# One step later for the weight work, earlier halves at a block's start, and a reordered attention end

## The reference

```python
q_p, k_p = phi(q), phi(k)                 # exp(+-(proj - max|proj|)), 256 features
kv = einsum('bhsf,bhsd->bhfd', k_p, v);  z = k_p.sum(axis=2)
attn = (q_p @ kv) / (q_p @ z + 1e-6)      # x: 2304 x 512
h = x @ w_in                              # 512 -> 2048
y = (h * clip(h + 3, 0, 6) / 6) @ w_out   # 2048 -> 512
e = argmax(y @ w_gate)                    # one of 8 experts per row
out = p[e] * sigmoid(y @ w_output_gate)[e] * (relu(y @ w1[e]) @ w2[e])
```

## Time and profile before

| what | us |
|---|---|
| median of 3 runs | 891.78 (891.55 to 892.68) |
| profiled execution, whole | 891.2 |
| its span | 889.4 |
| PE busy | 842.6 (95%) |
| DVE busy | 573.2 (64%) |
| ACT busy | 411.7 (46%) |

### The profile page before, as it was taken

The page is one execution under the profiler, slowest core; times in us unless marked ns, Lnnn a source line. Parts: engine busy times, 40 slices in busy tenths (PEclk is TensorE's granted clock), DMA queues, the critical chain, the costliest instruction groups (busy, mean ns, idle before and its releaser), DMA issues.

```text
span 889.4 us, 19938 instructions
## 1 busy us (share of the span) xinstructions
PE 842.6 (95%) x7258; PEld 563.1 (63%) x7259; DVE 573.2 (64%) x1200; ACT 411.7 (46%) x838; POOL 181.8 (20%) x207
## 2 busy tenths in 40 slices
PE   7999999997699999999999999999999999999994
PEld 5888777875355455455455455455766777777773
DVE  4777888885596987888788788864652345222221
ACT  5676577774356566565575575553301112111110
POOL 4444367751000002001001001001021222111100
PEclk9999999999999999999999999999999999999998
DMA  7345664442356365456555556256336572646610
GB/s 219 107 160 171 216 185 150 157 136 84 123 213 213 143 213 226 166 197 220 190 190 225 189 190 225 95 207 231 108 113 233 222 284 64 234 184 221 239 62 13
DMA packets 44884, 156.13 MB, mean 176 GB/s; under 512 B 7894, under 2 KB 12246, under 8 KB 38160
## 3 DMA queue, kind: packets, MB, share of 16 engines
q1 hardware_dynamic: 38896, 138.33, 43.5%
q0 software_dynamic: 5760, 16.80, 5.4%
q10 hardware_dynamic: 160, 0.07, 0.0%
HBM read 109.44 MB, written 47.47 MB: 176 GB/s over the span
## 4 chain that ended last, share of the span: by engine, by line
PE 77%; DVE 10%; issue 5%; ACT 3%; POOL 2%; DMA 1%; another core or an unknown queue 1%; DVEq 0%; POOLq 0%; ACTq 0%
PE ps L854 19%; PE ps L843 16%; PE ps L950 13%; PE ps L938 12%; PE ps L757 4%; PE ps L702 3%; PE ps L729 2%; DVE arena L1228 2%; DVE u_mx L1439 2%; ACT arena L1052 1%; POOL arena L527 1%; PE ps L928 1%; DVE y_mx L1417 1%; PE ps L716 1%; DMA arena<-in_moe_w 1%
## 5 line engine op out<-in xcount | busy, mean ns | idle before, releaser
L843 PE MATMUL ps<-arena,w_in_sb 128*128 128x384 f16 x1152 | 201.0, 326 | 1.5 <-issue 1.5
L854 PE MATMUL ps<-w_out_sb,arena 128*128 128x512 f16 x576 | 172.3, 381 | 13.5 <-DVE stage L1527 12.7
L843 PEld LDWEIGHTS ps<-arena,w_in_sb 128*128 128x128 f16 x1152 | 110.7, 98 | 75.5 <-issue 2.0
L1205 ACT ACTIVATE x_sb<-ps 128x512 f16<-128x512 f32 x54 | 31.6, 596 | 204.3 <-PE ps L938 173.8
L938 PE MATMUL ps<-x_sb,arena 128*128 128x128 f16 x2112 | 122.0, 219 | 3.2 <-issue 3.2
L938 PEld LDWEIGHTS ps<-x_sb,arena 128*128 128x128 f16 x2112 | 119.4, 98 | 7.4 <-issue 3.8
L950 PE MATMUL ps<-arena,x_sb 128*128 128x512 f16 x528 | 118.0, 379 | 2.1 <-DVE x_sb L1618 2.1
L854 PE MATMUL ps<-w_out_sb,stage 128*128 128x512 f16 x288 | 109.7, 381 | 0.0
L1174 ACT ACTIVATE arena<-relu 128x384 f16<-128x384 f32 x96 | 50.2, 523 | 118.6 <-DVE relu L1522 117.3
L1052 ACT ACTIVATE arena<-ps,arena 128x128 f32<-128x128 f32 x288 | 79.4, 382 | 54.9 <-DVE arena L1230 51.9
L854 PEld LDWEIGHTS ps<-w_out_sb,arena 128*128 128x128 f16 x576 | 55.6, 98 | 74.0 <-issue 17.5
(11 more groups left out here) (210 smaller groups left out, 1003.0 us busy)
## 6 DMA issues: line engine op xcount, KB each, us to landing
arena<-split SPq DMA_DIRECT2D x36, 1024.0 KB
arena<-in_moe_w SPq DMA_DIRECT2D x16, 2048.0 KB, 13.1
split<-arena SPq DMA_DIRECT2D x16, 2048.0 KB, 7.4
arena<-in_qkt SPq DMA_DIRECT2D x15, 576.0 KB, 6.2
stage<-in_moe_w_in SPq DMA_DIRECT2D x16, 512.0 KB, 4.3
stage<-in_moe_w_out SPq DMA_DIRECT2D x16, 512.0 KB, 5.4
x_sb<-rows POOLq DMA_DIRECT2D x27, 257.0 KB, 3.0
arena<-in_v SPq DMA_DIRECT2D x32, 128.0 KB, 4.6
```

The source lines that it names most:

```text
L843: last = nc.tensor.matmul(ps[:, HB[f % GB], 0:BN], w_in_sb[:, lw, c, f * P:(f + 1) * P], xt[:, a, c, lx, :], start=c == 0 and lw + lx == 0 ...
L854: last = nc.tensor.matmul(ps[:, YB + r, :], g_sb[lg_][:, f % GB, r * P:(r + 1) * P], w_out_sb[:, lw, f, :], start=f == 0 and lg_ + lw == 0 ...
```

## The change

It has four parts.

1. **Units one step later** (`UNIT_AT = 1`): every piece of a unit moves from step f to f + 1 on DVE and ACT. The second `unit_lo` of a block's third unit, which was in step 15, falls into step 0 of the next block.
2. **Block start.** DVE takes `row_scales` ahead of `gate_chunk(0)`, not behind `gate_lo(0)`; `gate_lo(1)` comes straight behind `gate_chunk(1)`; `rows_hi` moves from step 1 to 0 and `rows_lo` from step 3 to step 1. `Y_AT` goes from 4 to 3, and the transposes, copies, logits, ranks and routing go one step earlier with it.
3. **Attention end.** PE takes numerators 0 and 1 and the tails ahead of all four row transposes. `x_hi(0)` waits only for the scale it uses, `x_lo(0)` stands ahead of the two `piece_lo_of`, and the pieces of the last pair (with `wg_lo` and `base`) move behind the first gate of block 0. PE's wait for `x_ready` moves from ahead of `hidden(1)` to ahead of `output(0)`.
4. **POOL** does one `partition_all_reduce` into an unused tile `warm` at the end of attention.

```diff
-Y_AT, X_AT = 4, 10
+Y_AT, X_AT = 3, 10
+UNIT_AT = 1
+X_UP = 11
@@ POOL, last_pair
                 piece_hi_of(PAIRS - 1, 1)
+                nc.gpsimd.partition_all_reduce(warm[:], ones[:, 0:1], P, RMAX)
@@ PE, both
                     pe.wait_ge(pk_ready, u * 3 + 3)
-                    for c in range(2):
-                        x_transpose(0, c, X0[c])
...
                 else:
-                    for c in range(2, DC):
+                    for c in range(DC):
                         x_transpose(0, c, X0[c])
@@ PE, mlp_block
                 hidden(n, a, 0)
-                if first:
-                    pe.wait_ge(x_ready, PAIRS)
                 hidden(n, a, 1)
...
+                    if first and f == 0:
+                        pe.wait_ge(x_ready, PAIRS)
...
-                    if post and f == 9 - ahead:
+                    if post and f == Y_AT + 5 - ahead:
                         y_logits(n - 1)
@@ ACT, x_hi
-                    act.wait_ge(x_scale, 1)
+                    act.wait_ge(scale_step, X_UP)
@@ ACT, mlp_block
-                    k, j = divmod(f, 5)
-                    if k < units and j == 3:
+                    if post and f == 0:
+                        rows_hi(n - 1)
+                    k, j = divmod(f - UNIT_AT, 5)
+                    if 0 <= k < units and j == 3:
                         unit_hi(n * 3 + k, (odd + k) % 2, 0)
-                    if k < units and j == 4:
+                    if 0 <= k < units and j == 4:
                         unit_hi(n * 3 + k, (odd + k) % 2, 2)
-                    if post and f == 1:
-                        rows_hi(n - 1)
                     if post and Y_AT + 2 <= f + ahead // 2 < Y_AT + 2 + DC:
                         copy_yt(n - 1, f + ahead // 2 - Y_AT - 2, XB)
@@ DVE, values_pair and last_pair
                 x_scales()
+                x_lo(0)
                 for w in range(2):
                     piece_lo_of(u, a, w)
...
             def last_pair():
-                x_lo(0)
                 pair_out(PAIRS - 1, 1)
+
+            def last_pieces():
                 for w in range(2):
                     piece_lo_of(PAIRS - 1, 1, w)
@@ DVE, mlp_block
                 for f in range(FC):
-                    gate_chunk(n, f)
-                    if f in (0, FC - 1):
-                        gate_lo(n, f)
                     if post and f == 0:
                         row_scales(n - 1)
-                    k, j = divmod(f, 5)
+                    gate_chunk(n, f)
+                    if f in (0, 1, FC - 1):
+                        gate_lo(n, f)
+                    if f == 0 and not post:
+                        last_pieces()
+                    if f == 0 and post:
+                        unit_lo(n * 3 - 1, 1 - a, 2)
+                    if post and f == 1:
+                        rows_lo(n - 1)
+                    k, j = divmod(f - UNIT_AT, 5)
...
-                    if post and f == 3:
-                        rows_lo(n - 1)
-                    if f == 8 and units == 3:
+                    if f == 9 and units == 3:
                         x_lo(n + 1)
```

More of the change, by code:

```diff
@@ L174, in moe_program @@
         u_all = sb("u_all", [P, 2])
+        warm = sb("warm", [P, 1])
         u_pow = sb("u_pow", [P, UNITS])
@@ L914, in mlp_block @@
                         y_transpose(n - 1, f + ahead // 2 - Y_AT, XB)
-                    if post and f == 9 - ahead:
+                    if post and f == Y_AT + 5 - ahead:
                         y_logits(n - 1)
-                    if post and f == 11 - ahead:
+                    if post and f == Y_AT + 7 - ahead:
                         ranks(n - 1)
@@ L1166, in mlp_block @@
                     if isinstance(n, int) and n == 0 and f == 0:
+                        act.wait_ge(x_scale, 1)
                         act.wait_ge(pads_stored, 16 * E)
@@ L1174, in mlp_block @@
                     nc.scalar.mul(g_sb[0][:, f % GB, :], relu3[:, f % GB, :], CG / 6.0).then_inc(g_hi, 1)
-                    k, j = divmod(f, 5)
-                    if k < units and j == 3:
+                    if post and f == 0:
+                        rows_hi(n - 1)
+                    k, j = divmod(f - UNIT_AT, 5)
+                    if 0 <= k < units and j == 3:
                         unit_hi(n * 3 + k, (odd + k) % 2, 0)
-                    if k < units and j == 4:
+                    if 0 <= k < units and j == 4:
                         unit_hi(n * 3 + k, (odd + k) % 2, 2)
-                    if post and f == 1:
-                        rows_hi(n - 1)
                     if post and Y_AT + 2 <= f + ahead // 2 < Y_AT + 2 + DC:
                         copy_yt(n - 1, f + ahead // 2 - Y_AT - 2, XB)
-                    if post and f == 12 - ahead:
+                    if post and f == Y_AT + 8 - ahead:
                         gate_exp(n - 1)
@@ L1370, in last_pair @@
                                                op0=ALU.mult, op1=ALU.subtract).then_inc(wg_lo, 1)
+                dve.wait_ge(consts_made, 2)
+                nc.vector.tensor_copy(base[:, 0, :], start8[:]).then_inc(route, 1)
             def x_max():
@@ L1377, in x_scales @@
                 scales(slice(3, 4))
+                assert scale_steps[0] == X_UP + 1
                 scaled(nc.vector.tensor_tensor(s_h[:], s_inv[:, 3:4], s_inv[:, 0:1], ALU.mult))
@@ L1400, in _ @@
             last_pair()
-            dve.wait_ge(consts_made, 2)
-            nc.vector.tensor_copy(base[:, 0, :], start8[:]).then_inc(route, 1)
             def row_scales(n):
@@ L1566, in mlp_block @@
                 for f in range(FC):
-                    gate_chunk(n, f)
-                    if f in (0, FC - 1):
-                        gate_lo(n, f)
                     if post and f == 0:
                         row_scales(n - 1)
-                    k, j = divmod(f, 5)
+                    gate_chunk(n, f)
[8 more added lines that the diff above has]
+                    k, j = divmod(f - UNIT_AT, 5)
                     if j == 0 and 0 < k <= units:
                         unit_lo(n * 3 + (k - 1), (a + k - 1) % 2, 2)
-                    if j == 1 and k < units:
+                    if j == 1 and 0 <= k < units:
                         unit_search(n * 3 + k, (a + k) % 2, 0)
-                    if j == 2 and k < units:
+                    if j == 2 and 0 <= k < units:
                         unit_search(n * 3 + k, (a + k) % 2, 2)
-                    if j == 3 and k < units:
+                    if j == 3 and 0 <= k < units:
                         unit_scale(n * 3 + k, (a + k) % 2)
-                    if j == 4 and k < units:
+                    if j == 4 and 0 <= k < units:
                         unit_lo(n * 3 + k, (a + k) % 2, 0)
-                    if post and f == 3:
-                        rows_lo(n - 1)
-                    if f == 8 and units == 3:
+                    if f == 9 and units == 3:
                         x_lo(n + 1)
@@ L1588, in mlp_block @@
                         star_pick()
-                    if post and f == 11 - ahead:
+                    if post and f == Y_AT + 7 - ahead:
                         route_first(n - 1)
-                    if post and f == 13 - ahead:
+                    if post and f == Y_AT + 9 - ahead:
                         route_second(n - 1)
-                    if ahead and f == 13 - ahead:
+                    if ahead and f == Y_AT + 9 - ahead:
                         early_rows()
-                    if f not in (0, FC - 1):
+                    if f not in (0, 1, FC - 1):
                         gate_lo(n, f)
```

## The result

The changed kernel takes 881.72 us (median of 4 runs, 880.84 to 882.41) against 892.23 us for the kernel before in the same comparison (4 runs, 891.55 to 893.27): the ratio is 0.9881 with a 95% interval of 0.9864 to 0.9898, 1.2% faster. The forecast was 884.2, the range 878.0 to 889.0.

What follows compares the result with a forecast made beforehand. PE, busy 95% of the span, was taken to bound the kernel. Terms -4.4 - 8.8 + 3 x 1.2 + 0.5 + 1.7 = -7.4 from 891.2 gave 883.8, with 0.6 for the median 884.3, rounded to 884.2; range 878.0 to 889.0.

Steps and rivals of the forecast that it cites:

- Attention's end, -4.4: Attention's end: PE idles some 0.8 us instead of 4.39, hidden(0) begins at 209.1 instead of 213.53; -4.4 us.
- The bound that the clock might fall behind the short idle stretch: Attention's end: clock 0.59 behind the 0.8 us idle would add 1.1 to the first numerators and 0.6 to the transposes.
- Block 0, -8.8: Block 0: of 9.0 us of waits and low clock, all but 0.26 goes; -8.8 us.
- Blocks 1, 2 and 4, +1.2 each: DVE wait moves from step 1 to 2, gain nil; PE stands 1.2 us for ACT's copy at the transposes.
- The two waits named as signs, 1.3 and about 1.2: Blocks 1, 2 and 4: 1.3 us at output(2) for the gate, about 1.2 at the transposes for ACT's copy.
- The rival that the waits vanish: Blocks 1 to 5: DVE's queue keeps up, 5.7 us of waits go, no copy is late; 872.9 us, chance 0.12.
- Its halfway case, 878.6: Blocks 1 to 5: copy in time but T(2), output of step 2, still late; 878.6 us, counted within the 0.12 chance.
- Block 3, +0.5: Block 3, behind the loop's back branch: its wait of 0.4 goes, the copy is 0.9 late; +0.5 us.
- block 5, +1.7: Block 5, transposes one step earlier: copy of group 0 late 1.25, the next 0.2, the start 0.2; +1.7 us.
- Experts, 0: Behind block 5: last unit stored and first expert's loads some 5 us later, costed at nothing.
- The sum: All terms together: -7.4 us against the profiled execution's 891.2, giving 883.8, before 0.6 for the median.
- 2.5 us in each of four blocks: Slower-than-before rival: copy_xt of group 3 late behind unit_hi in step 15, delaying the next block's hidden(0); 893.8 us, chance 0.05.

Runs made afterwards that it cites:

- experiment 1: The kernel before plus only the unused partition reduction on POOL at attention's end: 888.90 us, ratio 0.9958.
- experiment 3: The changed kernel without the unused partition reduction on POOL: 887.44 us, ratio 0.9945 to the kernel before.
- experiment 5: The kernel before with only the MLP blocks' new order (units one step later, early block start), no attention-end change, no unused reduction: 893.40 us, ratio 1.0019.
- Experiment 4: The changed kernel with the copy of the transposed rows placed ahead of the unit's high half on ACT: 878.26 us, ratio 0.9839.
- experiment 2: The kernel before with only the attention-end part of the change: 887.11 us, ratio 0.9947.
- experiment 6: The changed kernel with rows_lo back in step 3 and the transposes one step later (Y_AT = 4): 880.38 us, ratio 0.9874.
- experiment 7: The changed kernel with rows_hi in step 1, rows_lo in step 4, transposes two steps later (one step earlier each in block 5): 879.05 us, ratio 0.9860.
- experiment 8: The changed kernel run once more, unmodified, for the spread: 881.58 us, ratio 0.9889.
- Experiment 9: The copy-first version (experiment 4) with gate_lo ahead of the search in step 2 too: 880.14 us, ratio 0.9867.
- experiment 10: The copy-first version (experiment 4) with gate_lo ahead of the search in steps 2 and 3: 883.08 us, ratio 0.9903.
- experiment 11: The copy-first version (experiment 4) with gate_lo directly behind its chunk in all sixteen steps: 925.31 us, ratio 1.0357.

## Why the prediction was right

**Attention's end, -4.4.** Between the two traces it is -4.27, and by the same steps: `x_hi` 200.96 to 202.55, numerators from 203.13, transposes from 205.68, 0.22 for bank 3, hidden(0) at 209.26 (forecast 209.1). But the near match is in part luck. Measured from the z sums the term is -4.87, so the forecast was 0.47 short, and a start 0.60 later, which the change did not make, covers that up. The bound that the clock might fall behind the short idle stretch did not come in: it was granted in full.

**Block 0, -8.8.** Measured -8.61. The load is issued at 211.24 and used at 220.40 (211.0 and 220.0 in the forecast), output(2) waits 0.29 (0.26), and POOL's gap moved in front of the unused reduction. That is 6.8 us of waits and 1.8 of lower clock. Experiments 1, 3 and 5 split this term: the reordering removes the wait for the load, the unused reduction the gap, and each leaves the other's wait standing.

**Blocks 1, 2 and 4, +1.2 each.** Measured +1.19, +0.96 (with a back branch that was 0.21 shorter) and +1.17. The layout of the queue held: output(0), (1) and (2) begin 6.14, 10.04 and 15.21 us behind hidden(0), against 5.99, 9.98 and 15.17. The copy of the transposes runs from 25.54 to 26.32 against 25.5 to 26.3. The two waits named as signs, 1.3 and about 1.2, stand in the rows as 1.12 and 0.93; the forecast counted from an undisturbed start, and the rows count PE's idle time alone. Experiment 4 removes the stall at the copy and nothing else, and the five blocks become 4.4 us shorter in spite of a back branch that was 0.9 longer; experiment 5 shows the reordering as a loss. The rival that the waits vanish (872.9) is refuted by both. Its halfway case, 878.6, is what the kernel gives once the copy is put first: 878.26.

**Block 3, +0.5, and block 5, +1.7.** Measured -0.15 and +1.43. The copy is 0.93 late in block 3, as laid out, but a 0.74 us issue wait of PE ahead of output(0), which the trace of before has in this block, is absent after. The three traces with the old order of the steps have such a wait there (0.74, and 1.02 and 1.28 in experiments 1 and 2), and none of those with the new order has. I had not read that row: this term was 0.65 too high.

**Experts, 0.** Measured -1.02. The code there is the same. Before has one wait of 2.1 us for `x_sb` (L1618) there, after has one of 1.2 for an expert's load. In the traces of experiments 1 to 10 the phase took 261.3 to 263.9 us, so a microsecond either way is scatter of this stretch and need not be the change's doing; which transfer decides it in a given execution I did not settle.

**The sum.** -7.4 was forecast and -9.3 measured between the two traces: 1.0 is the expert phase, 0.65 block 3, 0.5 attention's end, 0.3 block 5, 0.2 the back branch, against 0.6 for the later start of the z sums and 0.2 for block 0. The median lies another 0.7 below the forecast, since 0.6 was added for a median above the profiled execution, and after the change the two agree (881.72 and 881.79). No step of the forecast failed; mostly the terms put at nothing or by analogy were off. One rival has a slip: 2.5 us in each of four blocks, added to the forecast of 884.3, is 894.3 and not 893.8, which starts from the profiled execution.

The expectations of experiments 6, 7, 10 and 11 fared worse than the forecast, and mostly for one reason. The forecast time of each followed the queue of DVE with care and took ACT's to be free, though the rivals of 10 and 11 named ACT or a lack of slack. In block 1 of the changed kernel DVE's low halves of gates 1 to 3 end 0.1 to 0.7 us ahead of the outputs that need them, and ACT's copy is 0.93 late, so what is taken out of one queue appears in the other. Experiment 9 had the wait right (1.1 expected, 1.26 measured) and the time 1.8 us too low.

## What to carry to other kernels

Price a moved step on both engines that feed the critical one, from the start of the block, instruction by instruction: if the reordered queue holds as much work ahead of the same deadline, the wait only changes its place. Here the wait for DVE moved by one step at no gain, and a second one, for ACT, cost about 1.2 us in each of blocks 1, 2 and 4. Of two instructions in one step, the one that another engine waits for goes first; that change of order was worth 3.5 us, where the reordering of the steps in blocks 1 to 5 had cost 4.6. And where an engine's first instruction of a kind is preceded by a long idle gap that no semaphore explains, an unused one placed in an idle stretch takes the gap off the path: 3.4 us alone, 5.7 once it was the last long wait of its block and took the low clock with it.

## What the runs showed of the hardware

In all thirteen traces POOL's first partition reduction began 5.5 to 6.3 us behind the two instructions that set POOL up for it, in its old place (5.8 in the kernel before, 6.3 in experiment 3) and in its new one (5.8 in the changed kernel, 5.7 in experiment 1), and every later one within half a microsecond of its maxima. The Trainium skill, GPSIMD Engine Reference, section 2.1, says that the first call of a freshly loaded kernel pays a load of about 6 us. These rows agree. They also show that an unused call on a one-column tile is enough to pay it.

The back branch of the loop over blocks held PE between 1.2 and 2.3 us in all profiled executions but that of the slowest version (0.16), with the same loop in each. In four of them it was 2.11, 2.12, 2.15 and 2.26 us. Behind 2.12 (experiment 6) and 2.26 (experiment 9) the granted clock fell to its lower level of 1.2 GHz; the windows of experiment 9:

```profile
412.20:416.20 4.00, 4.00 (x15) 2.02 (x16) 1.49 (x7) 0.23 (x1) 0.00 (x0) 0.58 0.01 4
416.20:419.80 3.60, 3.60 (x24) 2.15 (x22) 2.54 (x4) 2.98 (x6) 0.00 (x0) 1.00 0.02 5
```

The 36 matmuls of hidden(0) to (2) took 7.65 us there (7.70 in experiment 6) instead of 6.02, which the executions with 2.11 (experiment 10) and 2.15 (experiment 4) kept. So 1.6 us of what experiments 6 and 9 failed to gain in their traces is the clock and not their order, and waits of this length do or don't cost PE a second time. In experiment 11 the granted clock was 0.53 from 345.70 to 349.20, behind a wait of 2.02, and stayed full behind the three other waits of that length; behind all three waits of 3.2 us it fell.
